# The last matrix product of a three-stage network: half of its K by Strassen's seven products, written transposed

## Chip, cores and metric

The kernel runs on one core of one Trainium2 chip. The metric is the device time of one execution in microseconds (us).

## What is computed

An attention over 2 x 12 heads of 448 tokens, then a two-layer network with a leaky ReLU, then a gated network behind a root-mean-square norm, all in float32:

```python
scores = cap * tanh(q @ k.T / 8 / cap);  attn = softmax(scores);  x = attn @ v    # 2 x 12 x 448 x 64 -> x: 896 x 768
h = x @ w_in;  g = maximum(0.01 * h, h);  x = g @ w_out                            # 768 -> 2048 -> 768
xn = x / sqrt(mean(x * x) + 1e-6) * rms_g
g = xn @ w_gate;  silu = g / (1 + exp(-g));  val = xn @ w_val                      # 768 -> 1536, twice
out = (silu * val) @ w_out2                                                         # 1536 -> 768
```

## The kernel before

Each float32 operand of the large products is split into an upper and a lower part (`hi`, `lo`, of type fp32r), and a product is three matmuls: hi by hi, hi by lo, lo by hi. ScalarE (ACT) copies the upper parts, GpSimd (POOL) or VectorE (DVE) subtracts to make the lower ones. All order is written out by hand, engine by engine, with semaphores; each engine works through its own list and stands still when the head of the list waits.

**Strassen units.** The gate and value products run as 12 units, `s = U1` to `UNITS - 1` (8 to 19), one for each 128 of the 1536 hidden features. A unit computes a 2 x 2 block product (gate and value rows by the two halves of K, times K halves by the two batches) as seven products P1, P5, P7, P6, P3, P2, P4 of 9 matmuls each (`product`, L1345 to L1360: 3 tiles of K by 3 matmuls of 128 x 448), 63 in all. The operands of tokens (`x_hi`, `x_lo`, seven blocks B11, T1, T3, T2, B22, B21, T4 of three tiles) stay for all units. For every weight panel ACT makes `w_hi` (L632), POOL `w_lo` (L518), in a ring of seven slots, so that panel n waits until PE has used panel n - 7. DVE adds weight panels up for P5, P7, P6, P3 (`s_part`, L933 to L942).

**Around PE in a unit.** P3 goes on in the bank of P5, and so waits until DVE has taken P5 out of it (`take_p5`, L955, semaphore `a_done`). `take_p5` adds to P1, which ACT has copied out (`keep_p1`, L638, `p1_kept`). P4 goes on in the bank of P7 and waits for `take_p7` (L961, `a2_done`), P2 waits for `p1_kept`. The rest of the unit on DVE: `take_p6` L965, `value_22` L1162, `gate_sum` L1168, `gate_12` L1172, `gate_11` L1177, `value_21` L1181, and `weighted` (L1188 and L1191), which writes the two tiles of `act_full` (features x tokens, 12 x 2 tiles of 128 x 448). ACT does silu between (L801).

**Last product before.** 504 matmuls at L1516 (`token_tile`): the stationary operand is a 128 x 128 piece of `act_full`, split into `split_hi` and `split_lo` for each of 7 tiles of tokens, the moving one is a row block of `w_out2` (`v2_hi`, `v2_lo`), 384 columns wide (512 and 256 for the last tile). Panels `v2` are split ahead: four during units 13 to 18, the other eight in unit 19 and after. DVE and ACT scale the results (L1262, L854) and SP stores them.

Of the kernel before, what the change touches and what calls it, by code (L numbers as in the profile page):

```python
# [17 lines left out]
def build(nc, qk, v, cap, w_in, w_out, w_gate, w_val, w_out2, rms_g, out, recips):  # L18
    PAIRS, _, QK = qk.shape
    S = out.shape[0] // 2  # L20
# [20 lines left out]
    P1, P5, P7, P6, P3, P2, P4 = range(7)  # L41
# [4 lines left out]
    UNITS = U1 + N2  # L46

# [22 lines left out]
    pe_order += list(range(W_OUT, widx(UNITS, 0)))  # L70
    count = {n: i + 1 for i, n in enumerate(pe_order)}
    assert len(count) == widx(UNITS, 0)

    with ExitStack() as ctx:
# [24 lines left out]
        u2 = [buf(f"u2_{s}", S, F32) for s in range(2)]  # L99
        extra = buf("extra", S, F32)  # L100
        r_bc = buf("r_bc", B * S, F32)
        sq_acc = buf("sq_acc", B * S, F32)
# [28 lines left out]
        EARLY = 4  # L131
        v2_hi, v2_lo, v2_raw = [], [], []
        for where in (RING, SPARE):
            at(where)
            for _ in range(EARLY // 2):
                v2_hi.append(buf(f"v2_hi{len(v2_hi)}", DM, F32R))
                here = place["at"]
                v2_raw.append(buf(f"v2_raw{len(v2_raw)}", DM, F32))
                at(here)
                v2_lo.append(buf(f"v2_lo{len(v2_lo)}", DM, F32R))  # L140
        split_hi, split_lo = [], []
        for where, late, split, part in ((XH, v2_hi, split_hi, "hi"), (XL, v2_lo, split_lo, "lo")):
            at(where)
            split.append(buf(f"split0_{part}", N2 * 128, F32R))
            for k in range(EARLY, N2):
                late.append(buf(f"v2_{part}{k}", DM, F32R))
            split.append(buf(f"split1_{part}", N2 * 128, F32R))
# [19 lines left out]
        v2_in = [sem(f"v2_in{s}") for s in range(EARLY)]  # L167
# [58 lines left out]
        v2_hi_done = sem("v2_hi_done")  # L226
        v2_lo_pool = sem("v2_lo_pool")
        v2_lo_dve = sem("v2_lo_dve")
        v2_lo_half = sem("v2_lo_half")
        split_hi_done = sem("split_hi_done")  # L230
        split_lo_done = sem("split_lo_done")
        rows_done = sem("rows_done")
        evac_act = sem("evac_act")
        evac_dve = sem("evac_dve")
# [112 lines left out]
        def v2_block(k):  # L347

            return (N2 * 128 + (k - EARLY + 1) * DM - 1) // (KH * S)

        def split_block(tt):
            return (N2 * 128 - 1 + tt * (N2 * 128 + (N2 - EARLY) * DM)) // (KH * S)


        v2_pool = list(range(EARLY)) + list(range(EARLY, N2, 2))
        v2_dve = list(range(EARLY + 1, N2, 2))

        def wait_v2_lo(eng, k):
            if k in v2_pool:
                eng.wait_ge(v2_lo_pool, v2_pool.index(k) + 1)  # L360
            else:
                eng.wait_ge(v2_lo_dve, v2_dve.index(k) + 1)

        def pieces_of(tt):
            return [(0, 11), (11, 12)] if tt == 0 else [(0, N2)]

        def pieces_done(tt):
            return sum(len(pieces_of(t)) for t in range(tt))


        def half_cols(tt, half):
            cut = HALF if tt < TT - 1 else 512
            return slice(cut * half, cut if half == 0 else DM)

        def staging(tt, half):
            return (p1 + a_t)[(2 * tt + half) % 4][:, 0:HALF] if tt < TT - 1 else r_bc[:, half_cols(tt, half)]

        def row_bank(tt, half):
            c = half_cols(tt, half)
            return ps[:, (4 + 2 * tt + half) % 8, 0:c.stop - c.start]  # L380

        def unit_of(n):

            if n < W_OUT:
                return n // 7, n % 7
            return U1 + (n - W_GV) // 7, (n - W_GV) % 7

        def w_source(n):

            if W_OUT <= n < W_GV:  # L390
                k = n - W_OUT
                return w_raw[(RAW_OUT + k // 2) % 4][:, cols(k % 2, HALF)]
            s, j = unit_of(n)
            if j in (P1, P2):
# [5 lines left out]
        def v2_source(k):  # L400
            return v2_raw[k][:, :] if k < EARLY else w_raw[(RAW_V2 + k - EARLY) % 4][:, :]
# [5 lines left out]
        def _(sp):  # L407
# [32 lines left out]
            def raw_free(r):  # L440
# [63 lines left out]

        @block.gpsimd
        def _(pool):
# [73 lines left out]
            def value_lo(k):  # L580
                pool.wait_ge(v2_hi_done, k + 1)
                pool.tensor_tensor(v2_lo[k][:, :], v2_source(k), v2_hi[k][:, :].bitcast(F32), ALU.subtract).then_inc(v2_lo_pool, 1)

            def value_lo_half(k, half):
                pool.wait_ge(v2_hi_done, k + 1)
                c = cols(half, HALF)
                lower = pool.tensor_tensor(v2_lo[k][:, c], v2_source(k)[:, c], v2_hi[k][:, c].bitcast(F32), ALU.subtract)
                if half == 1:
                    lower.then_inc(v2_lo_pool, 1)
                else:  # L590
                    lower.then_inc(v2_lo_half, 1)
# [1011 lines left out]
```

## Time and profile before

| | |
|---|---|
| time, median of 3 runs | 575.03 us (574.76 to 576.02) |
| profiled execution: its own time | 574.06 us |
| its span, first to last instruction | 572.3 us |
| PE busy | 567.6 us, 99% |
| weight loads (PEld), DVE, ACT, POOL busy | 493.5, 357.0, 277.6, 271.9 us |
| granted TensorE clock | 1.000 of 2.4 GHz |

1.8 us of the profiled execution's time lie outside its span. PE's busy time counts overlapping matmuls once, so that it says that matmuls follow each other without a gap, not that each is as short as it could be. The rows below are in us from the start of the span.

### The profile page before, as it was taken

To read this page: it belongs to the slowest core of one execution; us is meant where nothing else is said; L and a number is where in the kernel's file an instruction comes from. 1 tells how busy PE (TensorE), PEld (TensorE's weight loads), DVE (VectorE), ACT (ScalarE), POOL (GpSimd) and SP (SyncE) were. 2 spreads that over 40 slices of the span, in tenths; PEclk is the share of its full clock that TensorE was granted. 3 is DMA by queue.
4 is the path that set the end of the run, shared out by engine and by line. 5 is a ranking of instruction groups with operands and counts; after the bars stand their busy time and mean duration, and the time that the engine had idled before them with its cause. 6 is when DMAs were issued, how large, how long until landed. Compare 5 with 4: busy or idle time off the path is not lost.

```text
span 572.3 us, 7765 instructions
## 1 busy us (share of the span) xinstructions
PE 567.6 (99%) x2823; PEld 493.5 (86%) x2823; DVE 357.0 (62%) x484; ACT 277.6 (49%) x453; POOL 271.9 (48%) x236
## 2 busy tenths in 40 slices
PE   8999999999999999999999999999999999999998
PEld 5555655799999999999999999999999999999997
DVE  4479897685555455326974699988788878511120
ACT  6889888236544454437533555333445435311110
POOL 1036373569665633226643487755688855000000
PEclk9999999999999999999999999999999999999999
DMA  6355432213112222120210011611111114000001
GB/s 170 95 173 164 116 102 65 43 49 111 57 55 67 98 85 57 55 56 27 84 55 29 2 55 57 218 58 56 57 56 55 56 60 162 29 27 29 29 27 56
DMA packets 30006, 41.49 MB, mean 73 GB/s; under 512 B 17040, under 2 KB 18832, under 8 KB 29968
## 3 DMA queue, kind: packets, MB, share of 16 engines
q1 hardware_dynamic: 29824, 40.99, 22.9%
q8 instruction: 23, 0.38, 0.3%
q14 instruction: 15, 0.12, 0.1%
q10 hardware_dynamic: 144, 0.00, 0.0%
HBM read 38.15 MB, written 2.80 MB: 72 GB/s over the span
## 4 chain that ended last, share of the span: by engine, by line
PE 98%; DMA 1%; DVE 1%; issue 0%; DVEq 0%
PE ps L1358 45%; PE ps L1425 21%; PE ps L1516 15%; PE ps L1295 10%; PE ps L1283 4%; PE ps L1301 2%; PE ps L1287 2%; DMA qk_raw<-in_qk 1%; PE ps L1477 0%; PE ps L1500 0%; DVE qk_lo L986 0%; DVE qk_lo L991 0%; DVE r_bc L1262 0%; DVE qk_hi L984 0%; DVE capc L999 0%
## 5 line engine op out<-in xcount | busy, mean ns | idle before, releaser
L518 POOL TENSOR_TENSOR w_lo<-w_raw,w_hi 128x384 fp32r<-128x384 f32 x92 | 107.2, 1169 | 133.8 <-ACT w_hi L632 133.5
L1358 PE MATMUL ps<-x_hi,w_hi 128*128 128x448 f32 x420 | 154.2, 367 | 0.0
L1358 PE MATMUL ps<-x_hi,w_lo 128*128 128x448 f32 x420 | 153.4, 365 | 0.0
L1358 PE MATMUL ps<-x_lo,w_hi 128*128 128x448 f32 x420 | 153.4, 365 | 0.0
L518 POOL TENSOR_TENSOR w_lo<-s_sum,w_hi 128x384 fp32r<-128x384 f32 x80 | 89.1, 1121 | 45.1 <-ACT w_hi L632 44.9
L1358 PEld LDWEIGHTS ps<-x_hi,w_hi 128*128 128x128 f32 x420 | 78.9, 188 | 7.6 <-issue 1.1
L1358 PEld LDWEIGHTS ps<-x_hi,w_lo 128*128 128x128 f32 x420 | 78.9, 188 | 6.3
L1358 PEld LDWEIGHTS ps<-x_lo,w_hi 128*128 128x128 f32 x420 | 78.9, 188 | 6.1
L632 ACT ACTIVATE w_hi<-s_sum 128x384 fp32r<-128x384 f32 x80 | 41.6, 523 | 76.9 <-PE ps L1358 67.9
L1295 PE MATMUL ps<-probs,v_ones 128*128 128x448 f32 x144 | 56.8, 542 | 0.0
L632 ACT ACTIVATE w_hi<-w_raw 128x384 fp32r<-128x384 f32 x92 | 47.3, 515 | 7.5 <-PE ps L1358 7.0
L608 ACT ACTIVATE probs<-ps,capc 128x896 f32<-128x896 f32 (+1 forms) x48 | 42.1, 903 | 12.2 <-PE ps L1283 9.7
L1295 PEld LDWEIGHTS ps<-probs,v_ones 128*128 128x128 f32 x144 | 27.0, 189 | 23.1 <-issue 22.6
L1516 PE MATMUL ps<-v_hi,split_lo 128*128 128x384 f32 (+2 forms) x168 | 44.9, 336 | 0.0
L1516 PE MATMUL ps<-v_lo,split_hi 128*128 128x384 f32 (+2 forms) x168 | 44.9, 336 | 0.0
L1516 PE MATMUL ps<-v_hi,split_hi 128*128 128x384 f32 (+2 forms) x168 | 44.9, 336 | 0.0
L615 ACT ACTIVATE probs<-probs,capc 128x1344 f32<-128x1344 f32 (+2 forms) x25 | 41.1, 1643 | 0.8
L1043 DVE TENSOR_TENSOR x_lo<-g,x_hi 128x448 fp32r<-128x448 f32 x32 | 22.1, 737 | 23.7 <-ACT x_hi L664 23.7
L1043 DVE TENSOR_TENSOR ring_lo<-g,ring_hi 128x448 fp32r<-128x448 f32 x32 | 24.6, 813 | 15.2 <-ACT ring_hi L664 15.2
L1516 PEld LDWEIGHTS ps<-v_hi,split_hi 128*128 128x128 f32 x168 | 30.6, 188 | 0.6
L1516 PEld LDWEIGHTS ps<-v_hi,split_lo 128*128 128x128 f32 x168 | 30.6, 188 | 0.5
L1516 PEld LDWEIGHTS ps<-v_lo,split_hi 128*128 128x128 f32 x168 | 30.6, 188 | 0.5
(145 smaller groups left out, 915.8 us busy)
## 6 DMA issues: line engine op xcount, KB each, us to landing
w_raw<-in_w_out SPq DMA_DIRECT2D x24, 384.0 KB, 3.1
w_raw<-in_w_in SPq DMA_DIRECT2D x16, 384.0 KB, 3.6
qk_raw<-in_qk SPq DMA_DIRECT2D x11, 480.0 KB, 4.2
w_raw<-in_w_gate SPq DMA_DIRECT2D x12, 384.0 KB, 3.0
w_raw<-in_w_val SPq DMA_DIRECT2D x12, 384.0 KB, 3.7
v_ones<-in_v SPq DMA_DIRECT2D x12, 224.0 KB, 3.3
recip_row<-recips SPq DMA_DIRECT2D x12, 224.0 KB, 3.4
v_raw<-in_w_out SPq DMA_DIRECT2D x4, 384.0 KB, 6.4
```

The lines of the kernel that those rows point to most:

```text
L518: pool.tensor_tensor(w_lo[:, c], source, w_hi[:, c].bitcast(F32), ALU.subtract).then_inc(w_lo_done, 1)
L608: act.activation(tiles(probs_of(p, i, n), S), ps[:, bank_of(p, i):bank_of(p, i) + n, 0:S], ACT.Tanh, scale=capc[:, 4:5]).then_inc(tanh_don ...
L615: act.activation(c, c, ACT.Exp, scale=capc[:, 2:3], bias=capc[:, 6:7]).then_inc(exp_done, 1)
L632: act.activation(w_hi[:, c], w_source(n), ACT.Copy).then_inc(w_hi_done, 1)
L1043: dve.tensor_tensor(ring(i, b, ring_lo, x_lo), g_tile(2 * f + b), ring(i, b, ring_hi, x_hi).bitcast(F32), ALU.subtract).then_inc(g_lo_done, 1)
L1283: last = pe.matmul(ps[:, bank + h, 0:S], k[HEAD[h], k_c], q[HEAD[h], 0:S], start=(k is hi and q is hi), stop=(k is lo))
L1287: last = pe.matmul(ps[:, bank, 0:S], k[:, k_c], q[:, 0:S], start=(k is hi and q is hi), stop=(k is lo))
L1295: pe.matmul(ps[:, pv_bank(p) + h, 0:S], v_ones[p % 2][:, c:c + 128], probs[p % 2][:, (2 * t + h) * S:(2 * t + h + 1) * S], start=(t == 0), ...
L1301: last = pe.matmul(ps[:, pv_bank(p) + h, 0:S], v_ones[p % 2][HEAD[h], c:c + 128], probs[p % 2][HEAD[h], 2 * MAIN * S:(2 * MAIN + 1) * S], ...
L1358: last = pe.matmul(ps[:, base(s) + BANK_OF[j], 0:S], w[:, w_c], x[:, xs(j, c)], start=(j in (P1, P5, P7, P6) and c == 0 and w is w_hi and ...
L1425: last = pe.matmul(ps[:, ROW_BANK[m] + b, 0:S], w[:, w_c], ring(i, b, beside, in_x), start=(f == 0 and w is w_hi and x == "hi"), stop=(f = ...
L1516: last = pe.matmul(row_bank(tt, half), a[:, c], w[f][:, half_cols(tt, half)], start=(f == 0 and a is hi and w is v2_hi), stop=(f == N2 - 1 ...
```

## The change

1. The last product is computed transposed: the stationary operand is now a panel of `w_out2`, the moving one a tile of `act_full` (448 tokens), the result 768 x 896, and the host turns it. It runs as three units, s = 20, 21, 22, each for two of the six row tiles.
2. In a unit, the first half of K (hidden tiles 0 to 5, `F0 = 6`) is multiplied plainly: 2 rows x 2 batches x 6 tiles x 3 = 72 matmuls (`plain`, four panels PA to PD). The second half (tiles 6 to 11) goes by Strassen's seven products, 63 matmuls. A unit has 135 matmuls and 11 weight panels, three units have 405. Both parts add into the same four banks.
3. Strassen on the token side needs seven blocks of three tiles of activations, made by new code: `z_t1`, `z_t3`, `z_t2`, `z_t4` (sums on DVE), `z_hi` on ACT, `z_lo` on DVE; T1 (for P5) in tiles of its own (`t1_upper`, `t1_lower`), made in units 14 to 19. The splits of the 12 plain tiles are spread over units 11 to 19 (`PLAIN_SPLITS`, `plain_upper` on ACT, `plain_lower_half` on POOL). z tiles and weight panels are begun in unit 19.
4. Results are put together on DVE in two steps each (`result_22`, `_12`, `_11`, `_21`: an addition from the bank, then a multiplication with `r_bc`) and stored as 128 x 448 tiles.
5. In the attention, the product of probabilities and values (`weigh_tile`, `weigh_rest`) loads 65 columns of `v_ones` in place of 128 and writes 65 partitions; DVE reads 65 as before.

```diff
@@ attention
-                    pe.matmul(ps[:, pv_bank(p) + h, 0:S], v_ones[p % 2][:, c:c + 128],
+                    pe.matmul(ps[0:D + 1, pv_bank(p) + h, 0:S], v_ones[p % 2][:, c:c + D + 1],
...
@@ PE: bank_free, the last product
+                if s >= UNITS and j == P1:
+                    pe.wait_ge(u2_done, s - 1)
+                    pe.wait_ge(c22_done, s - 1)
+                elif s >= UNITS and j == P6:
+                    pe.wait_ge(p1_kept, s + 1)
...
+            def plain(s, row, b, half):
...
+                if half == 0:
+                    if (row, b) == (0, 0):
...
+                    elif (row, b) == (0, 1):
+                        pe.wait_ge(a_done, s + 1)
+                    elif (row, b) == (1, 0):
+                        pe.wait_ge(a2_done, s + 1)
+                    else:
+                        pe.wait_ge(u2_done, s + 1)
...
+            for s in range(UNITS, LAST):
+                product(s, P1)
+                product(s, P5)
+                plain(s, 0, 0, 0)
+                plain(s, 0, 0, 1)
+                plain(s, 0, 1, 0)
+                product(s, P7)
+                plain(s, 0, 1, 1)
+                plain(s, 1, 0, 0)
+                product(s, P6)
+                plain(s, 1, 0, 1)
+                plain(s, 1, 1, 0)
+                plain(s, 1, 1, 1)
+                for j in (P3, P2, P4):
+                    product(s, j)
@@ ACT, from unit 19 on
+            s = UNITS
+            keep_p1(s - 1)
+            last_weights(s, P1)
+            t1_upper(2)
+            z_upper(B11)
+            last_weights(s, P5)
+            z_hi(T3, 0)
+            z_hi(T3, 1)
+            last_weights(s, PA, PB)
+            silu(s - 1, 1)
+            last_weights(s, P7)
+            z_hi(T3, 2)
+            silu(s - 1, 0)
+            last_weights(s, PC)
+            z_upper(T2)
+            last_weights(s, P6, PD)
+            keep_p1(s)
...
@@ DVE, end of unit 18, unit 19 and after
+                if s - U1 - F0 in (0, 2, 4):
+                    z_t1((s - U1 - F0) // 2)
+                if s - U1 - F0 in (2, 4):
+                    t1_lower((s - U1 - F0) // 2 - 1)
...
+            def z_t2(c):
+                dve.wait_ge(t3_done, c + 1)
+                dve.wait_ge(z_lo_done, z_count[B11, c])
+                dve.tensor_tensor(z_tile(T2, c), z_tile(T3, c), z_tile(B11, c), ALU.add).then_inc(t2_done, 1)
...
+            def result_21(s):
+                dve.wait_ge(prod_done, count[widx(s, P4)])
+                dve.tensor_tensor(u2[s % 2][:, :], bank(s, BANK_D), u2[s % 2][:, :], ALU.add).then_inc(c21_done, 1)
+                dve.wait_ge(c21_done, s + 1)
+                dve.tensor_tensor(u2[s % 2][:, :], u2[s % 2][:, :], r_bc[:, cols(0)], ALU.mult).then_inc(o_done, 1)
```

What moves is shown by the order of instructions in the built programs. In the rows, `a_t_61` is `a_t[1]`, `u_1_63` is `u2[1]`, `p_0_58` is `p1[0]`, `t_tile` and `t_lo` are T1's tiles, `w_raw_51` a loaded weight panel; line numbers are those of each program.

DVE before, the end of unit 18 (the two `weighted` lines) and the first half of unit 19:

```order
L1188 TENSOR_TENSOR act_full<-a_t_60,sq_68 128x448
L1191 TENSOR_TENSOR act_full<-u_0_62,sq_67 128x448
L955 TENSOR_TENSOR a_t_61<-ps,p_1_59 128x448
L961 TENSOR_TENSOR a_t_61<-ps,a_t_61 128x448
L1201 TENSOR_TENSOR split_lo<-act_full,split_hi 128x1408
L965 TENSOR_TENSOR u_1_63<-ps,p_1_59 128x448
```

DVE in the change, the same place (L1244 is `z_t1`, L1248 `t1_lower`, L1253 `z_t3`, L1267 `z_lo`, L972 and L975 `s_part`, L996 `take_p5`, L1002 `take_p7`):

```order
L1236 TENSOR_TENSOR act_full<-u_0_62,sq_67 128x448
L1244 TENSOR_TENSOR t_tile<-act_full 128x448
L1248 TENSOR_TENSOR t_lo<-t_tile,t_hi_103 128x448
L972 TENSOR_TENSOR s_sum<-w_raw_52 128x384
L975 TENSOR_TENSOR s_sum<-w_raw_51,w_raw_52 128x384
L996 TENSOR_TENSOR a_t_61<-ps,p_1_59 128x448
L1253 TENSOR_TENSOR act_full<-act_full 128x448 x2
L1248 TENSOR_TENSOR t_lo<-t_tile,t_hi_104 128x448
L1267 TENSOR_TENSOR x_lo<-act_full,x_hi 128x448
L1002 TENSOR_TENSOR a_t_61<-ps,a_t_61 128x448
L1267 TENSOR_TENSOR x_lo<-act_full,x_hi 128x448 x2
L1008 TENSOR_TENSOR u_1_63<-ps,p_1_59 128x448
```

Between unit 18's last instruction and `take_p5` of unit 19 there were none and are now four; between `take_p5` and `take_p7` there were none and are four.

DVE in the change, the second half of unit 19 up to `take_p5` of unit 20, the last row (L1211 is `gate_sum`, L1215 `gate_12`, L1230 and L1236 `weighted`, L1258 `z_t2`); before, no instruction of this kind followed, only two pieces of splitting:

```order
L1211 TENSOR_TENSOR sq_68<-ps,u_1_63 128x448
L1215 TENSOR_TENSOR sq_68<-sq_68,r_bc 128x448
L1267 TENSOR_TENSOR x_lo<-act_full,x_hi 128x448
L1230 TENSOR_TENSOR act_full<-a_t_61,sq_68 128x448
L1253 TENSOR_TENSOR act_full<-act_full 128x448
L1220 TENSOR_TENSOR sq_67<-ps,r_bc 128x448
L978 TENSOR_TENSOR s_sum<-s_sum,w_raw_51 128x384
L1267 TENSOR_TENSOR x_lo<-act_full,x_hi 128x448
L1224 TENSOR_TENSOR u_1_63<-ps,u_1_63 128x448
L1236 TENSOR_TENSOR act_full<-u_1_63,sq_67 128x448
L1258 TENSOR_TENSOR act_full<-act_full 128x448 x3
L981 TENSOR_TENSOR s_sum<-w_raw_51,s_sum 128x384
```

From unit 18's last instruction to the third `z_t2` DVE has two instructions of T1's, then 26 of unit 19's list; L996 of unit 20 stands right behind the last row.

ACT in the change, from the second silu of unit 19 to `keep_p1` of unit 20 and beyond (L835 is `z_hi`, L648 `weight_hi`, L656 `keep_p1`):

```order
L819 ACTIVATE sq_67<-sq_67 128x448
L648 ACTIVATE w_hi<-w_raw_54 128x384
L835 ACTIVATE x_hi<-act_full 128x448 x3
L648 ACTIVATE w_hi<-s_sum 128x384
L648 ACTIVATE w_hi<-w_raw_54 128x384
L656 ACTIVATE p_0_58<-ps 128x448
L835 ACTIVATE x_hi<-act_full 128x448 x6
```

The copy of P1 of unit 20 (L656) stands behind the three upper parts of T2, which wait for `z_t2` on DVE. Before, there was no such copy after unit 19's.

## Rows read from the trace of the kernel before

**Rows 1.** The page: busy shares, and slices of the span.

```profile
PE 567.6 (99%) x2823; PEld 493.5 (86%) x2823; DVE 357.0 (62%) x484; ACT 277.6 (49%) x453; POOL 271.9 (48%) x236
...
PE   8999999999999999999999999999999999999998
...
DVE  4479897685555455326974699988788878511120
...
POOL 1036373569665633226643487755688855000000
PEclk9999999999999999999999999999999999999999
```

**Rows 2.** Chain that ended last, 300 to 573: start, length, what.

```profile
348.29 133.16 PE ps L1358 x657
481.45 88.11 PE ps L1516 x504
```

**Rows 3.** DVE's groups, 360 to 470: busy us, mean ns, idle before.

```profile
L1191 DVE TENSOR_TENSOR act_full<-u,sq 128x448 f32<-128x448 f32 x9 | 13.0, 1441 | 0.0
L1172 DVE TENSOR_TENSOR sq<-sq,r_bc 128x448 f32<-128x448 f32 x9 | 11.6, 1292 | 0.3
L936 DVE TENSOR_TENSOR s_sum<-w_raw,w_raw 128x384 f32<-128x384 f32 x8 | 11.1, 1382 | 0.0
L939 DVE TENSOR_TENSOR s_sum<-s_sum,w_raw 128x384 f32<-128x384 f32 x9 | 8.3, 925 | 0.0
L942 DVE TENSOR_TENSOR s_sum<-w_raw,s_sum 128x384 f32<-128x384 f32 x9 | 7.8, 869 | 1.3 <-DVE s_sum L939 0.5
...
L1188 DVE TENSOR_TENSOR act_full<-a_t,sq 128x448 f32<-128x448 f32 x9 | 5.5, 617 | 0.0
...
L933 DVE TENSOR_TENSOR s_sum<-w_raw 128x384 f32<-128x384 f32 x8 | 4.4, 546 | 0.0
```

**Rows 4.** DVE's instructions in order of time: start, length, which.

```profile
450.62 0.61 DVE L965 TENSOR_TENSOR u<-ps,p 128x448 f32<-128x448 f32 x1
451.15 0.61 DVE L1162 TENSOR_TENSOR a_t<-ps,a_t 128x448 f32<-128x448 f32 x1
452.39 0.63 DVE L1168 TENSOR_TENSOR sq<-ps,u 128x448 f32<-128x448 f32 x1 [0.64 <-PE ps L1358]
453.06 1.34 DVE L1172 TENSOR_TENSOR sq<-sq,r_bc 128x448 f32<-128x448 f32 x1
...
458.39 0.55 DVE L933 TENSOR_TENSOR s_sum<-w_raw 128x384 f32<-128x384 f32 x1
458.86 1.38 DVE L936 TENSOR_TENSOR s_sum<-w_raw,w_raw 128x384 f32<-128x384 f32 x1
460.16 0.61 DVE L955 TENSOR_TENSOR a_t<-ps,p 128x448 f32<-128x448 f32 x1
...
469.79 1.44 DVE L1191 TENSOR_TENSOR act_full<-u,sq 128x448 f32<-128x448 f32 x1
```

**Rows 5.** POOL's instructions in order of time.

```profile
458.81 1.01 POOL L518 TENSOR_TENSOR w_lo<-w_raw,w_hi 128x384 fp32r<-128x384 f32 x1 [0.82 <-ACT w_hi L632]
```

**Rows 6.** ACT's instructions in order of time.

```profile
457.77 0.55 ACT L638 ACTIVATE p<-ps 128x448 f32<-128x448 f32 x1 [1.30 <-PE ps L1358]
458.21 0.52 ACT L632 ACTIVATE w_hi<-w_raw 128x384 fp32r<-128x384 f32 x1
```

**Rows 7.** Start of the last product, on PE.

```profile
481.28 0.52 PE L1516 MATMUL ps<-v_hi,split_hi 128*128 128x384 f32 x2
```

**Rows 8.** The end: last matmul, last scaling, last store.

```profile
569.26 0.28 PE L1516 MATMUL ps<-v_hi,split_lo 128*128 128x256 f32 x1
569.58 0.48 DVE L1262 TENSOR_SCALAR r_bc<-ps,rms 128x256 f32<-128x256 f32 x1 [11.97 <-PE ps L1516]
570.09 0.33 SPq L500 DMA_DIRECT2D out<-r_bc  x1
```

**Rows 9.** All stores of the output.

```profile
DMA to landing us min/median/max: 1.7/2.0/3.7
```

**Rows 10.** Chain, 40 to 60: products with the values, one of 12 pairs.

```profile
44.98 4.51 PE ps L1295 x12
49.49 0.95 PE ps L1301 x4
```

**Rows 11.** Weight loads of these products: duration ns min/median/max.

```profile
L1301 PEld LDWEIGHTS ps<-probs,v_ones x48: 182/184/186, 16.6 to 104.3; 64*128 64x128 f32 x48
```

**Rows 12.** The same for L1295.

```profile
L1295 PEld LDWEIGHTS ps<-probs,v_ones x144: 186/190/191, 9.2 to 103.4; 128*128 128x128 f32 x144
```

More of the change, by code:

```diff
@@ L19, in build @@
     PAIRS, _, QK = qk.shape
-    S = out.shape[0] // 2
+    S = out.shape[1] // 2
     B, D, T = 2, 64, 4
@@ L129, in build @@
         SPARE = place["at"]
[L131 to L147, printed above, removed]
+        at(G)
+        act_lo = buf("act_lo", N2 * B * S, F32R)
+        at(RING)
+        plain_ring = buf("plain_ring", 8 * S, F32R)
+        at(SPARE)
+        plain_spare = buf("plain_spare", 4 * S, F32R)
+        T1_AT = place["at"]
+        t1_tile = buf("t1_tile", KH * S, F32)
+        at(T1_AT)
+        t1_lo = buf("t1_lo", KH * S, F32R)
+        at(EXTRA)
+        t1_hi = [buf("t1_hi0", S, F32R)]
+        at(SQ_ACC)
+        t1_hi += [buf(f"t1_hi{k}", S, F32R) for k in (1, 2)]
         ps = ctx.enter_context(nc.psum_tensor("ps", [128, 8, 512], F32))
@@ L364, in pieces_of @@
[L364 to L380, printed above, removed]
+        PLAIN = [(k, b) for k in range(F0) for b in range(B)]
@@ new lines, in z_tile, with t1, z_parts, result @@
+        def z_tile(blk, c):
+            return {B22: act_tile(F0 + KH + c, 1), B21: act_tile(F0 + KH + c, 0), T3: act_tile(F0 + c, 1)}.get(blk, act_tile(F0 + c, 0))
+        def t1(k, c):
+            return k[:, cols(c)]
+        def z_parts(*blks):
+            return [(blk, c) for blk in blks for c in range(KH)]
+        z_all = z_parts(B11, T3, T2, B22, B21, T4)
+        z_count = {part: i + 1 for i, part in enumerate(z_all)}
+        def result(s, kind):
+            return ((1, 1, a_t[s % 2]), (0, 1, sq[1]), (0, 0, sq[0]), (1, 0, u2[s % 2]))[kind]
@@ L578, in _, with plain_lower_half @@
                 weight_lo(widx(U1 + 1, j))
[L580 to L591, printed above, removed]
+            def plain_lower_half(i):
+                k, b = PLAIN[i]
+                pool.wait_ge(plain_hi_done, i + 1)
+                pool.tensor_tensor(plain_lo(k, b), act_tile(k, b), plain_hi(k, b).bitcast(F32), ALU.subtract).then_inc(plain_lo_done, 1)
             for s in range(U1 + 2, UNITS):
@@ new lines, in _ @@
+                if s - U1 - F0 in (2, 4):
+                    t1_lower((s - U1 - F0) // 2 - 1)
+            s = UNITS - 1
+            s_part(s + 1, P5)
+            s_part(s + 1, P7)
+            take_p5(s)
+            z_t3(0)
+            z_t3(1)
+            t1_lower(2)
+            z_lo(B11, 0)
+            take_p7(s)
+            z_lo(B11, 1)
+            z_lo(B11, 2)
+            take_p6(s)
+            value_22(s)
+            z_lo(T3, 0)
+            gate_sum(s)
+            gate_12(s)
@@ new lines, in _ @@
+            z_lo(T3, 1)
+            weighted_1(s)
+            z_t3(2)
+            gate_11(s)
+            s_part(s + 1, P6)
+            z_lo(T3, 2)
+            value_21(s)
+            weighted_0(s)
+            for c in range(KH):
+                z_t2(c)
+            s_part(s + 1, P3)
+            s = UNITS
+            take_p5(s)
+            for c in range(KH):
+                z_lo(T2, c)
+            take_p7(s)
+            for c in range(KH):
+                z_t4(c)
+            for c in range(KH):
+                z_lo(B22, c)
@@ new lines, in _ @@
+            take_p6(s)
+            for blk in (B21, T4):
+                for c in range(KH):
+                    z_lo(blk, c)
+            result_22(s)
+            s_parts(s + 1)
+            result_12(s)
+            result_11(s)
+            result_21(s)
+            for s in range(UNITS + 1, LAST):
+                take_p5(s)
+                take_p7(s)
+                take_p6(s)
+                result_22(s)
+                if s + 1 < LAST:
+                    s_parts(s + 1)
+                result_12(s)
+                result_11(s)
+                result_21(s)
@@ L1589 @@
         "w_val": panels(inputs["moe2_w_val"]),
[L1590 removed]
+        "w_out2": panels(w_out2).reshape(dm // 128, 128, 2, f2 // 2).transpose(0, 2, 1, 3),
         "rms_g": inputs["moe2_rms_g"],
```

367 lines of the change are left out of this document (202 added, 165 removed).

## The prediction

> **What bounds the kernel now.** I began with the page's busy shares and slices [rows 1]. The reader is to see 99% on PE and a 9 in every slice but the first and the last, at a granted clock of 9 (full) throughout: no other engine ends anything for long. The chain that ended last confirms it [rows 2]: units 10 to 19 with the end of unit 9 are one unbroken piece of 657 matmuls in 133.16 us, 0.2027 us each, and the last product one piece of 504 in 88.11 us. So a matmul taken out is worth 0.2027 us, and anything that makes PE stand still is paid in full. DVE has 8s and 9s up to the last product and 0 to 2 in it, POOL 5 to 8 and then nothing [rows 1]: the change puts work on DVE where it was nearly full (units 18 and 19), so I read its list next [rows 3, 4].
>
> Two numbers set DVE's pace. An instruction on 448 columns starts 0.53 us after the one before (450.62, 451.15), one on 384 columns 0.47 (458.39, 458.86) [rows 4]. And an instruction with both inputs in SBUF takes much longer when POOL works: L1191 1.44 us where L1188, of the same form, takes 0.62; L936 1.38 where L933 takes 0.55 [rows 3]. L936 of 458.86 was issued while POOL's L518 ran from 458.81 for 1.01 us [rows 5], and the next instruction started at 460.16 [rows 4], 0.34 after POOL's end: DVE waited for POOL and then did its work. The five such lines of a unit lose 0.82, 0.68, 0.84, 0.38 and 0.32 us against 0.617 and 0.546 [rows 3], 0.61 on average.
> The Trainium skill (SBUF — State Buffer, Who interferes with whom) says that `tensor_tensor` with both inputs in SBUF contends with GpSimd's reads; by that rule the new DVE work, nearly all of this form, is the dearest kind to add beside POOL, and the trace agrees.
>
> **The change, part by part**, against the profiled execution (574.06 us, span 572.3); its time is 0.97 below the median of the runs, 575.03, and I add the difference to the median.
>
> *PE's work.* 504 matmuls become 405 of 448 columns. 405 x 0.2027 = 82.1, against 88.1 [rows 2]: -6.0.
>
> *Where PE waits.* In unit 20 PE does P1, P5 and two plain pieces, 36 matmuls, then needs `a_done`, since the next piece adds to the bank of P5. Unit 20 can start where the last product started, 481.28 [rows 7]; its B11 tiles must be there by then, for which see below. So PE asks for `a_done` at 481.28 + 36 x 0.2027 = 488.6. It is set by `take_p5` of unit 20, which waits for ACT's copy of P1, which stands behind the upper parts of T2, which wait for `z_t2` on DVE. The sum for DVE:
> - unit 18's last instruction ends at 469.79 + 1.44 = 471.2 [rows 4];
> - `z_t1` 0.53, `t1_lower` beside POOL's w_lo about 1.4 (as L1191): 473.1;
> - of unit 19's list 26 instructions to the third `z_t2`: 23 of 448 and 3 of 384 columns, 23 x 0.53 + 3 x 0.47 = 13.6;
> - POOL does six things meanwhile (w_lo of P5, PA, PB, P7, PC and the plain tile 11). Each meets a DVE instruction of the slow form; placing them one by one I get 3.9 in all, 0.65 each, near the average of 0.61. If they cost what these five lines lose spread over all seven panels, 3.04 / 7 = 0.43, it is 2.6; at the dearest line's 0.84, 5.0;
> - instructions that need the result just made start 0.14 later (452.39 to 453.06, where 0.53 would do [rows 4]), four times, with silu about 0.6.
> The third T2 tile is there at 473.1 + 13.6 + 3.9 + 0.6 = 491.2. ACT then copies its last T2 tile (0.44), two weight panels (0.41 each) and P1 (0.55, [rows 6]), `take_p5` takes 0.61 and semaphores about 0.2: 493.9. PE waits 5.3 us (4.0 to 6.4 by the bounds on POOL), and 0.1 to start again.
> Behind `take_p5` DVE has the lower parts of T2; PE wants P6 after 36 more matmuls, 7.3 us on, and they need 3 x 0.53 and one meeting with POOL. Nothing else is late.
>
> *Before unit 20.* `take_p5` of unit 19 ends about 474.6 (473.1 + 0.94 + 0.61); PE, which starts unit 19 at 481.28 - 63 x 0.2027 = 468.5, needs it at 468.5 + 36 x 0.2027 = 475.8. `take_p7` follows two `z_t3`, `t1_lower`, one `z_lo`, two meetings with POOL: about 478.9; P4 needs it at 479.4. The third B11 tile comes after `z_lo` twice more, 1.1 and two meetings: about 481.2; its matmuls come at 481.28 + 6 x 0.2027 = 482.5. So these cost nothing, with 0.5 us to spare at the tightest. If the DVE is later by d, it is d on the whole and not twice, since the 5.3 would shrink by what PE lost before.
>
> *Plain splits and panels.* Twelve ACT copies of 0.44 in nine units where ACT is half idle, and POOL's in place of the `v2` panels it did there: not on the path. The loads are as many bytes as before and a unit ahead. In units 21 and 22 DVE has at most 15 instructions in 135 x 0.2027 = 27.4 us, ACT and POOL 11 panels: PE does not wait. Should a store be late, `take_p5` and `take_p6` of unit 22 wait for one issued a unit before; it lands in 2.0 to 3.7 [rows 9]: covered by 20 us.
>
> *The end.* Before, 2.76 us from the last matmul's end (569.26 + 0.28) to the end of the span. Now: 0.04, addition 0.67 to the next start, multiplication 0.61, issue 0.03, landing 2.0 (the median of 192 KB stores in place of 1.7 for the 128 KB one) [rows 8, 9], and the 0.5 after it: 3.85. +1.1.
>
> *The 65 columns.* L1295 takes 0.376 a record, 12 in 4.51, and L1301's 4 take 0.95 where two such pairs would be 0.75 [rows 10]: up to 0.2 us of weight load is exposed for each of 12 pairs, 2.4 in all. A load of 64 rows takes 184 ns, of 128 rows 190 [rows 11, 12]: rows don't matter, and no row has fewer columns. Bounds: 0 and half of 2.4, -1.2. I take -0.3, nearer to nothing, since the loads' length moved so little with size.
> The Trainium skill (TensorE: Matmul & The Clock Gate, LDWEIGHTS) gives a load as P / 1.2 ns for P columns, rows aside: 107 ns becomes 54, which over 12 to 24 exposed loads is an estimate of 0.6 to 1.3 us, so that the sum would be 0.3 to 1.0 lower than with mine. That rows matter little the trace shows; columns no run here shows.
>
> Sum: -6.0 + 5.3 + 0.1 + 1.1 - 0.3 = +0.2. 574.3 for such an execution, 575.2 as a median.
>
> **Rivals.**
> 1. *POOL costs DVE more* (slower). Place: unit 19's list on DVE. One more meeting is +0.84 at the dearest [rows 3], and at 5.0 in all the wait is 6.4: 575.2 + 1.1 = 576.3; with one more, or with 65 columns worth nothing, 577.2. It decides from +1.0 on DVE's chain. For: every line added to DVE is of the slow form. Against: POOL has long idle times here. 0.28.
> 2. *DVE is quicker than I add up* (faster). With 2.6 for POOL the wait is 4.0, and with -1.2 for the columns 573.0. For: two T1 tiles and the lower parts may fall where POOL stands idle. Against: the five lines of before meet POOL in every unit. 0.15.
> 3. *PE is fed throughout* (faster): the preparation begun a unit sooner does what it says. Then 575.03 - 6.0 + 1.1 - 0.3 = 569.8. It needs the P1 copy 5.3 us sooner, as with eight of DVE's 26 instructions not ahead of it; the order shows all 26. 0.05.
> 4. *The columns are worth it* and the rest is as summed: 574.3, within 0.2% still; in the forecast's case.
>
> **How the numbers follow.** 0.2% is 1.15 us, about what a measurement of this kernel can tell from no change. The forecast's case, 574.0 to 576.2, has 0.52. Rival 1 is slower in nearly all of its 0.28. Rival 2 gives 573.0 to 573.9, rival 3 less: faster 0.20. The range reaches over rivals 1 and 2, 572.9 to 577.4, and leaves out rival 3.
>
> **What would show it.** In the profile of the changed kernel: 405 matmuls in the last product at 0.203 each; one gap on PE of 5 us some 36 matmuls into it, released by `take_p5` (L996), that by ACT's L656, that by DVE's L1258; DVE without a gap from 470 to 491; the slow form at 1.0 to 1.6 us beside POOL; 3.9 us from the last matmul to the end; L1301's four records at 0.85 to 0.95. I am wrong if the gap is under 4 or over 6.5, if PE waits elsewhere in units 19 to 22, or if the products with the values move by over 1.2 us.

## The result, and the profile after

The changed kernel takes 577.89 us (577.45 to 578.95), the kernel before beside it 575.29: 1.0047 times as long, 95% interval 1.0031 to 1.0062. Forecast were 575.2 us and a range up to 577.4. It is slower by 2.6 us, and outside the range.

The profiled execution took 578.34 us, with a span of 576.5. First the page's busy shares and slices, to lay beside [rows 1]:

```profile
PE 565.0 (98%) x2724; PEld 475.6 (82%) x2724; DVE 390.3 (68%) x543; ACT 287.1 (50%) x495; POOL 308.0 (53%) x269
...
PE   8999999999999999999999999999999999699997
...
DVE  4479896595654354336974799988888999681513
...
PEclk9999999999999999999999999999999999899999
```

PE has 99 matmuls fewer, as forecast, and one slice with a 6; in the same slice the granted clock shows an 8, where the kernel before had a 9 throughout. The chain that ended last has the same place in detail (start, length, what):

```profile
349.72 120.40 PE ps L1509 x594
...
491.26 0.62 DVE act_full L1258
...
491.96 0.49 ACT x_hi L835
...
493.94 0.49 ACT w_hi L648
494.44 0.44 ACT p L656
494.87 0.02 issue
494.90 0.64 DVE a_t L996
495.53 0.04 issue
495.58 3.62 PE ps L1686 x9
499.19 1.85 PE ps L1509 x9
501.05 3.69 PE ps L1686 x18
```

Read upward from 495.58, this is the chain that the prediction wrote down: `take_p5` (L996) releases PE, the copy of P1 (L656) releases `take_p5`, and ahead of the copy stand two weight panels and the upper parts of T2, which had waited for `z_t2` (L1258). Read downward, there is something the prediction doesn't have: the nine matmuls behind the stand-still take 3.62 us, while the same form takes 3.69 for eighteen a little later. PE's matmuls in order of time, with the time stood still in brackets:

```profile
489.87 0.37 PE L1686 MATMUL ps<-plain_spare,w_lo 128*128 128x448 f32 x1
495.58 0.74 PE L1686 MATMUL ps<-plain_ring,w_hi 128*128 128x448 f32 x1 [5.34 <-DVE a_t L996]
496.12 0.57 PE L1686 MATMUL ps<-act_lo,w_hi 128*128 128x448 f32 x1
496.49 0.57 PE L1686 MATMUL ps<-plain_ring,w_lo 128*128 128x448 f32 x1
...
498.73 0.46 PE L1686 MATMUL ps<-plain_ring,w_lo 128*128 128x448 f32 x1
499.03 0.36 PE L1509 MATMUL ps<-x_hi,w_hi 128*128 128x448 f32 x1
499.23 0.37 PE L1509 MATMUL ps<-x_lo,w_hi 128*128 128x448 f32 x1
```

From start to start the gap is 5.71 us, of which 0.205 is the matmul's own: PE stands 5.5 us. Behind it the starts lie 0.37 us apart (496.12, 496.49), and 0.20 from 499.03 on. Nine matmuls need 499.03 - 495.58 = 3.45 where they would need 9 x 0.205 = 1.85: 1.6 us more, below called the surcharge. The windows say why (columns: width of the window, busy time of PE with its count, granted clock, share of DMA, GB/s):

```profile
494.00:495.00 1.00, 0.00 (x0) 1.00 0.00 0
495.00:496.00 1.00, 0.42 (x1) 0.76 0.00 0
496.00:497.00 1.00, 1.00 (x4) 0.50 0.00 0
...
498.00:499.00 1.00, 1.00 (x4) 0.53 0.00 0
499.00:500.00 1.00, 1.00 (x6) 1.00 0.00 0
```

The granted clock was 1.00 (2.4 GHz), fell to 0.50 (1.2 GHz) just as PE had stood still for 5.5 us and began again, and was back at 1.00 by 499. The Trainium skill (TensorE: Matmul & The Clock Gate, Why this matters for your kernels) warns that a long enough gap between matmuls in the middle of a kernel puts the clock back to its lower level; by that rule the wait costs more than its own length, and the trace agrees, with 1.6 us on top of 5.5.

The end of the kernel, in order of time:

```profile
572.37 0.36 PE L1509 MATMUL ps<-x_hi,w_lo 128*128 128x448 f32 x1
572.76 0.62 DVE L1296 TENSOR_TENSOR u<-ps,u 128x448 f32<-128x448 f32 x1 [0.46 <-PE ps L1509]
573.42 0.62 DVE L1298 TENSOR_TENSOR u<-u,r_bc 128x448 f32<-128x448 f32 x1
574.07 0.33 SPq L514 DMA_DIRECT2D out<-u  x1
```

From the last matmul's start to the end of the span are 576.5 - 572.37 = 4.15 us, where [rows 8] with the span of 572.3 have 3.0. The weight loads of the products with the values, beside [rows 11, 12]:

```profile
L1432 PEld LDWEIGHTS ps<-probs,v_ones x144: 133/138/138, 9.2 to 103.3; 128*65 128x65 f32 x144
L1438 PEld LDWEIGHTS ps<-probs,v_ones x48: 130/132/134, 16.4 to 104.2; 64*65 64x65 f32 x48
```

**A yardstick for the runs.** Executions of one kernel lie up to 4 us apart (the kernel before: 573.72 to 577.93 in 34). Its three profiles have spans of 572.3, 573.5 and 573.2, and the whole of that difference lies ahead of the last product, whose first matmul starts at 481.28, 482.56 and 482.22. What the last product and the end take is the same in all three. So for each profile I take the span less the start of the last product's first matmul: 572.3 - 481.28 = 91.0 for the kernel before, in all three profiles; 576.5 - 482.71 = 93.8 for the changed one. The difference, 2.8, stands beside that of the medians, 2.6.

### The profile page after: what moved, and what is told of

Read it like the earlier page. It is cut to its first block, busy times and chain, and to the rows that moved or that the text cites. A ratio compares the mean times of both kernels' runs of the same rounds, so it can differ in the third digit from the quotient of the medians.

```text
span 576.5 us, 7775 instructions
## 1 busy us (share of the span) xinstructions
PE 565.0 (98%) x2724; PEld 475.6 (82%) x2724; DVE 390.3 (68%) x543; ACT 287.1 (50%) x495; POOL 308.0 (53%) x269
## 4 chain that ended last, share of the span: by engine, by line
PE 90%; DVE 6%; issue 2%; DMA 1%; ACT 0%; DVEq 0%; ACTq 0%
PE ps L1509 49%; PE ps L1576 20%; PE ps L1432 8%; PE ps L1686 7%; PE ps L1420 3%; PE ps L1438 2%; PE ps L1424 1%; DVE x_raw L911 1%; DMA qk_raw<-in_qk 1%; DVE act_full L1253 0%; DVE x_lo L1267 0%; DMA sums<-x_raw 0%; DVE s_sum L978 0%; DVE sums_eps L917 0%; DVE act_full L1236 0%
## 5 line engine op out<-in xcount | busy, mean ns | idle before, releaser
L538 POOL TENSOR_TENSOR w_lo<-w_raw,w_hi 128x384 fp32r<-128x384 f32 x113 | 131.5, 1169 | 160.9 <-ACT w_hi L648 160.4
L1509 PE MATMUL ps<-x_hi,w_hi 128*128 128x448 f32 x474 | 174.3, 368 | 0.0
L1509 PE MATMUL ps<-x_hi,w_lo 128*128 128x448 f32 x474 | 173.5, 366 | 0.0
L1509 PE MATMUL ps<-x_lo,w_hi 128*128 128x448 f32 x474 | 173.5, 366 | 0.0
L648 ACT ACTIVATE w_hi<-s_sum 128x384 fp32r<-128x384 f32 x92 | 47.8, 523 | 93.9 <-PE ps L1509 68.5
L648 ACT ACTIVATE w_hi<-w_raw 128x384 fp32r<-128x384 f32 x113 | 57.8, 515 | 38.1 <-PE ps L1686 20.7
L1432 PE MATMUL ps<-probs,v_ones 128*65 128x448 f32 x144 | 56.6, 541 | 0.4 <-DVE x_raw L911 0.4
L1432 PEld LDWEIGHTS ps<-probs,v_ones 128*65 128x65 f32 x144 | 19.3, 137 | 30.6 <-issue 29.7
L981 DVE TENSOR_TENSOR s_sum<-w_raw,s_sum 128x384 f32<-128x384 f32 x23 | 25.9, 1124 | 2.5 <-DVE s_sum L978 0.5
L1576 PE MATMUL ps<-ring_hi,w_lo 128*128 128x448 f32 x96 | 27.5, 368 | 0.0
L1576 PE MATMUL ps<-ring_hi,w_hi 128*128 128x448 f32 x96 | 27.5, 367 | 0.0
L1576 PE MATMUL ps<-ring_lo,w_hi 128*128 128x448 f32 x96 | 27.5, 368 | 0.0
```

The lines of the kernel that those rows point to most:

```text
L538: pool.tensor_tensor(w_lo[:, c], source, w_hi[:, c].bitcast(F32), ALU.subtract).then_inc(w_lo_done, 1)
L648: act.activation(w_hi[:, c], w_source(n), ACT.Copy).then_inc(w_hi_done, 1)
L981: dve.tensor_tensor(dst, m1[:, upper], s_sum[:, cols(2, HALF)], ALU.subtract).then_inc(s_done, 1)
L1432: pe.matmul(ps[0:D + 1, pv_bank(p) + h, 0:S], v_ones[p % 2][:, c:c + D + 1], probs[p % 2][:, (2 * t + h) * S:(2 * t + h + 1) * S], start=( ...
L1509: last = pe.matmul(ps[:, base(s) + to, 0:S], w[:, w_c], x, start=(j in (P1, P5, P7, P6) and c == 0 and first), stop=(c == KH - 1 and w is ...
L1576: last = pe.matmul(ps[:, ROW_BANK[m] + b, 0:S], w[:, w_c], ring(i, b, beside, in_x), start=(f == 0 and w is w_hi and x == "hi"), stop=(f = ...
```

## The experiments

Theory: the wait at `a_done` in unit 20, and with it the half clock, turn a gain into a loss. Rivals: the half clock has another origin; the 65 columns or the stages ahead cost something; the end costs more.

**1. Both evacuations early.** ACT copies P1 of unit 20 ahead of unit 19's silu, and VectorE takes the fifth product after the third `z_t3`.

```diff
             last_weights(s, PA, PB)
+            keep_p1(s)
             silu(s - 1, 1)
...
             last_weights(s, P6, PD)
-            keep_p1(s)
...
             weighted_1(s)
             z_t3(2)
+            take_p5(s + 1)
             gate_11(s)
...
             s = UNITS
-            take_p5(s)
```

> The changed kernel with ACT's copy of P1 of unit 20 moved ahead of silu, and DVE's take_p5 of unit 20 moved behind the third z_t3 of unit 19. Theory A (PE's 5.5 us gap is the queue ahead of copy and take_p5, and the half clock of 3.4 us after it, worth 1.7, is a consequence of the gap): both go, 577.9 - 5.5 - 1.7 = 570.7 us, between 570 and 572, and no matmul at the lower clock. Theory B (DVE's whole list is the bound, whichever instruction PE waits for): the wait turns up one step later, at P6, for the lower parts of T2, and 575 us or more is left.

573.26 us, 0.9971 (0.9957 to 0.9986): faster than both kernels. The wait at `a_done` is gone, but two others are in its place:

```profile
496.45 0.44 PE L1686 MATMUL ps<-plain_ring,w_hi 128*128 128x448 f32 x1 [1.28 <-issue]
502.89 0.47 PE L1686 MATMUL ps<-plain_ring,w_hi 128*128 128x448 f32 x1 [0.66 <-DVE u L1008]
```

The matmuls ahead of them started at 494.80 and 501.86, so PE stands 1.45 and 0.83 us, for `take_p7` and `take_p6` of unit 20, which stand on VectorE behind the lower parts of T2 and B22. Their order is the same in the changed kernel, where the long wait and the slow matmuls behind it gave VectorE time for them. The granted clock of this stretch is 1.00, so these two stand-stills left it alone, and all ten executions have a mean of 0.998 to 1.0. The two waits, 2.3 us together, are nearly all of what the time lies above theory A's 570.7. Theory B put what is left at 575 or more, and at the lower parts themselves.

**2. The copy alone early**: of experiment 1 only the first part.

> Only ACT's copy of P1 moved, take_p5 stays behind the three z_t2 and one s_part on DVE. Theory A: a_done comes some 2 us sooner (take_p5 at about 492.7 instead of 494.9 in the profile), the gap is 3.5 us; 577.9 - 2.0 = 575.9 if the clock falls all the same, 574.2 if a gap of 3.5 us does not bring it down. Theory B: the same as theory A here.

576.36 us, 1.0024 (1.0007 to 1.0041), near the 575.9 that go with a fall of the clock. PE stands 3.9 us instead of 5.5 (491.53 to 495.65, start to start), but the clock falls sooner with respect to PE's restart:

```profile
493.00:494.00 1.00, 0.00 (x0) 1.00 0.00 0
494.00:495.00 1.00, 0.00 (x0) 0.68 0.00 0
495.00:496.00 1.00, 0.35 (x1) 0.50 0.00 0
...
501.00:502.00 1.00, 1.00 (x6) 0.91 0.00 0
```

Half clock lasts to 501, so more matmuls pay for it: in this execution the shorter wait has the larger surcharge, 2.6 us. It is the slowest of the ten, though (579.37 us). By the medians, 576.36 and 577.89, the copy alone is worth 1.5 us, about the 1.6 by which the wait got shorter, so on the whole the surcharge stayed.

**3. The wait filled.** In the changed kernel, 24 matmuls whose result is overwritten stand ahead of the waiting piece.

```diff
+                if s == UNITS:
+                    pe.wait_ge(c21_done, s - 1)
+                    for _ in range(24):
+                        pe.matmul(ps[:, base(s) + BANK_D, 0:S], w_hi[:, 0:128], t1_hi[0][:, :], start=True, stop=True)
                 plain(s, 0, 1, 0)
```

> The changed kernel with 24 matmuls of no use (448 columns, 24 x 0.203 = 4.9 us) on PE in the gap, into the bank that P7 starts anew afterwards; nothing else moved. Theory A (the clock falls because PE stands still): PE's real gap is under 1 us, the clock stays at its upper level, and the time is 577.9 - 1.7 = 576.2 us. Rival C (the plain matmuls after the gap are slow in themselves, by their operands or bank): 9 of them still take 0.37 us each, and 577.9 stays.

576.93 us, 1.0026 (1.0009 to 1.0043). The stretch on PE:

```profile
488.01 5.03 PE L1700 MATMUL ps<-t_hi,w_hi 128*128 128x448 f32 x24
493.57 0.47 PE L1686 MATMUL ps<-plain_ring,w_hi 128*128 128x448 f32 x1 [0.52 <-DVE a_t L996]
493.88 0.36 PE L1686 MATMUL ps<-act_lo,w_hi 128*128 128x448 f32 x1
494.08 0.37 PE L1686 MATMUL ps<-plain_ring,w_lo 128*128 128x448 f32 x1
```

Nothing useful is done sooner, the piece that waits for `a_done` starts 12.9 us after the last product began, as in the changed kernel, and yet the matmuls behind it start 0.20 apart, at a granted clock of 1.00. PE itself stands only 0.7 us. The yardstick gives 92.35 against 93.8. The medians, 576.93 and 577.89, are only 1.0 us apart and their intervals overlap. For the clock the run speaks by its profile and by the mean granted clock of all nine executions, 0.998 to 1.0; the changed kernel has 0.993 to 0.997 in each of its six.

**4. The 65 columns alone** in the kernel before.

```diff
-pe.matmul(ps[:, pv_bank(p) + h, 0:S], v_ones[p % 2][:, c:c + 128],
+pe.matmul(ps[0:D + 1, pv_bank(p) + h, 0:S], v_ones[p % 2][:, c:c + D + 1],
```

> The kernel before with the 65 columns alone. From the profile of the changed kernel, in which PE was 0.57 us ahead by 60 us and only 0.03 by 101: 575.0 to 575.3 us, nothing that can be measured. Rival: the saving stays and the time is 574.6 or less. It also shows whether the 1.6 us that units 2 to 7 took longer in the changed kernel's profile (0.2067 us a matmul in place of 0.2027) belong to this edit: then 576.5 or more.

575.35 us, 0.9996 (0.9982 to 1.0011): between -1.0 and +0.6 us, no effect that can be told from none, and the last product stays at 91.0.

**5. All three evacuations early.** From experiment 1, `take_p7` and `take_p6` of unit 20 come after the first lower part of T2 and of B22 instead of after the third.

```diff
-            for c in range(KH):
-                z_lo(T2, c)
+            z_lo(T2, 0)
             take_p7(s)
+            for c in range(1, KH):
+                z_lo(T2, c)
...
-            for c in range(KH):
-                z_lo(B22, c)
+            z_lo(B22, 0)
             take_p6(s)
+            for c in range(1, KH):
+                z_lo(B22, c)
```

> On top of both evacuations made early: in unit 20 VectorE takes the seventh product after the first T2 lower part instead of after the third, and the sixth after the first B22 lower part instead of after the third. The version before it still had TensorE standing 1.45 us at 494.8 (for the seventh product's evacuation, which ended at 496.35) and 0.83 us at 501.9 (for the sixth's, which ended at 502.84). Theory 1 (only these two waits are left): both go, 2.3 us less than 573.26, so 571.0 us (570.4 to 571.8), span 569.0, granted clock 1.0 before the tail. Rival (the split parts that are now 0.6 and 1.2 us later are waited for in their turn, by the products P6, P3, P2 or P4): one of the waits comes back further on, 572.3 to 573.3 us.

571.69 us, 0.9940 (0.9924 to 0.9956). One of the two waits is gone; of the other is left

```profile
502.55 0.48 PE L1688 MATMUL ps<-plain_ring,w_hi 128*128 128x448 f32 x1 [0.64 <-DVE u L1008]
```

with 0.8 us of stand-still (the matmul ahead started at 501.54). `take_p6` started at 501.88, although P6 had ended at about 500.3: it stood behind the B22 part, which ran from 500.53 for 1.43 us beside POOL.

**6. The kernel before, held up once.** GpSimd does five dependent operations on an idle buffer when token tile 2 is done, and PE waits for them before tile 3. Nothing else in the kernel waits.

```diff
+            pool.wait_ge(rows_done, 6)
+            for k in range(5):
+                at_least(pool, pause, k)
+                pool.tensor_tensor(extra[:, 0:HALF], extra[:, 0:HALF], extra[:, 0:HALF], ALU.mult).then_inc(pause, 1)
...
                 elif tt in (2, 3):
                     pe.wait_ge(act_done, 2 * N2)
+                    if tt == 3:
+                        pe.wait_ge(pause, 5)
```

> The kernel before, with TensorE held up once in its last product, between the third and the fourth token tile, by five dependent GpSimd operations on an idle buffer (1.06 us each plus about 0.2, so about 5.4 us); nothing else waits. Nothing is left out. Theory 1 (a stand-still of this length costs the stand-still and then a stretch at half the granted clock, 3.4 or 6.8 us of it, at 0.373 instead of 0.2027 us a matmul): 575.2 + 5.4 + 1.5 to 3.1 = 582.1 to 583.7 us, mean granted clock 0.993 to 0.997, and matmuls of twice the usual pitch right behind the gap. Rival (the half clock in the changed kernel came from something else in its place, not from the stand-still): 580.6 us, clock 1.0.

582.89 us, 1.0134 (1.0117 to 1.0151), a mean granted clock of 0.994 in all four executions, against 0.999 to 1.0 in the twelve of the kernel before. PE's matmuls (two to a row) around the stand-still:

```profile
519.58 0.51 PE L1521 MATMUL ps<-v_hi,split_lo 128*128 128x384 f32 x2
...
526.28 0.98 PE L1521 MATMUL ps<-v_hi,split_hi 128*128 128x384 f32 x2 [6.19 <-issue]
527.06 0.84 PE L1521 MATMUL ps<-v_lo,split_hi 128*128 128x384 f32 x2
527.70 0.84 PE L1521 MATMUL ps<-v_hi,split_lo 128*128 128x384 f32 x2
...
531.17 0.51 PE L1521 MATMUL ps<-v_hi,split_lo 128*128 128x384 f32 x2
```

The gap came out longer than planned, 6.53 us from start to start (the last matmul ahead of it started at 519.75). Behind it a matmul has 0.32 us (527.06, 527.70 for two) and from 531 on again 0.175. From the first to the last matmul of the product are 96.40 us against 87.98: 8.4, of which 6.35 stand-still and 2.05 surcharge. So the half clock comes from the stand-still and not from the changed kernel's work.

**7. The same with two operations.**

> The same with two GpSimd operations, a stand-still of about 2.3 us; nothing is left out. Stand-stills of 1.45 and 0.83 us left the clock alone in the version with both evacuations early, those of 3.9 and 5.5 us did not. Theory 1a (2.3 us is still free of a fall): 577.5 us, clock 1.0. Theory 1b (it falls here as well, in all or some executions): 578.5 to 580.6 us, clock 0.993 to 0.998.

577.70 us, 1.0051 (1.0033 to 1.0069). PE stands 2.1 us, the product is 2.13 longer, the granted clock 1.00 from before the pause to the last matmul; six of seven executions have a mean of 1.0, the seventh 0.997 and the longest time, 580.38. That one looks like a fall, though no profile shows it; at this length it is at most the exception.

**8. The changed kernel again.**

> The changed kernel itself once more, beside the others on the same chip. Theory 1: 577.9 us (577.3 to 578.5), every execution at a mean granted clock of 0.993 to 0.997, where the kernel before has 0.999 to 1.0. On the pitch of 0.2067 instead of 0.2027 us in units 2 to 7 (127 to 207 us: 388 matmuls where most profiles have 396): if it varies from execution to execution, this profile shows either; if it belongs to the changed kernel's program, it shows 388 again, and the kernel carries 1.6 us more that no step of the prediction has.

578.10 us, 1.0056 (1.0035 to 1.0077). All twelve timed executions of the changed kernel, these and the first six, have a mean clock of 0.993 to 0.997. The stand-still is 5.5 us again, but the clock fell earlier in it:

```profile
493.00:494.00 1.00, 0.00 (x0) 0.70 0.00 0
...
499.00:500.00 1.00, 1.00 (x4) 0.50 0.00 0
500.00:501.00 1.00, 1.00 (x6) 0.88 0.00 0
```

Here the surcharge is 90.25 - 89.65 = 0.6 us larger than in the first profile, 2.2 in all.

**9. P6 first.** From experiment 5, `take_p6` one operation sooner, ahead of the first B22 part.

```diff
-            z_lo(B22, 0)
             take_p6(s)
+            z_lo(B22, 0)
```

> As the version with all three evacuations early, with the sixth product of unit 20 taken one VectorE operation sooner, ahead of the first B22 lower part (1.43 us) instead of behind it. That version had one stand-still left, 0.81 us at 501.5, for the sixth product's evacuation, which began at 501.88 although the product had ended at about 500.3. Theory 1: the stand-still goes, 571.7 - 0.8 = 570.9 us (570.2 to 571.6). Rival (the B22 lower part that is now 0.6 us later is asked for at once by the product that follows): 571.7 us, with a gap at another line.

570.80 us, 0.9922 (0.9894 to 0.9951): 4.45 us faster than the kernel before. The chain has no wait from 400 to the end of the matmuls; its beginning:

```profile
399.99 85.95 PE ps L1511 x424
485.94 5.54 PE ps L1688 x27
491.48 1.82 PE ps L1511 x9
493.30 3.69 PE ps L1688 x18
496.99 1.82 PE ps L1511 x9
```

Its product, 82.51 us from first to last matmul, is what 405 matmuls take when nothing waits.

**10 to 12. Both kernels once more, two profiles of the one before and one of the changed.** Units 2 to 7, in the first layer of the network, differ between the two profiles, in a part that the change doesn't touch. The window 127 to 207 of the changed kernel (PE, PEld, DVE, ACT, POOL):

```profile
127.00:207.00 80.00, 80.00 (x388) 72.48 (x387) 42.45 (x62) 39.81 (x83) 51.90 (x48) 1.00 0.23 76
```

and of the kernel before:

```profile
127.00:207.00 80.00, 80.00 (x396) 73.93 (x395) 41.94 (x61) 41.33 (x87) 52.23 (x48) 1.00 0.24 80
```

Eight matmuls fewer, at a granted clock of 1.00 in both, are 1.6 us.

> The kernel before itself, one profile. In units 2 to 7 (127 to 207 us) two patterns of pitch have shown: 396 matmuls (mean 0.2027 us; the kernel before, and four others) or 388 (0.2067; the changed kernel twice, and three others). If it is a matter of the execution, either may show here; if of the program, 396 again. The last product lasts 87.98 us from its first to its last matmul in either case.

> The same once more: execution or program, as in the look ahead of it.

> The changed kernel, one more profile: 388 matmuls in 127 to 207 us for the third time if the slower pitch belongs to its program, 388 or 396 if it is a matter of the execution. Last product 89.5 to 90.5 us from its first to its last matmul, with a stand-still of 5.5 us at unit 20 and half the granted clock behind it.

575.34, 575.00 and 579.53 us. The changed kernel's third last product takes 89.95 us from first to last matmul, with a stand-still of 5.52 us and half the granted clock behind it, as expected. The kernel before has 395 or 396 in its three profiles, the changed one 388, 388 and 389. Of the others, experiments 1, 3, 4, 6 and 9 have 395 or 396, experiments 2, 5 and 7 have 388 or 389. Three and three look like a matter of the program. Against that stands that the timed executions don't show it: experiments 5 (388) and 9 (396) lie 0.9 us apart by their medians, and their last products alone differ by 83.41 - 82.51 = 0.9; experiment 7 (389) is 2.5 above the kernel before, its pause 2.1, where a slower pitch would add 1.6. And the profiled executions with 388 or 389 lie 0.45 to 3.0 us above the median of their kernel, all of them, those with 395 or 396 between 2.1 below and 0.5 above, as they would if it were a matter of the execution. What sets the pattern stays open. The result doesn't need it: see the sum below.

All of them by the yardstick (span less the start of the last product's first matmul, less the 91.0 of the kernel before), beside the difference of the medians:

| kernel | yardstick | difference | medians |
|---|---|---|---|
| changed | 576.5 - 482.71 = 93.8 | +2.8 | +2.6 |
| changed, again | 577.1 - 482.67 = 94.4 | +3.4 | +2.9 |
| 1, both early | 571.3 - 482.13 = 89.2 | -1.8 | -1.9 |
| 2, copy early | 577.6 - 484.37 = 93.2 | +2.2 | +1.2 |
| 3, filled | 573.0 - 480.65 = 92.35 | +1.35 | +1.7 |
| 4, 65 columns | 573.6 - 482.57 = 91.0 | 0.0 | +0.15 |
| 5, all early | 570.9 - 483.36 = 87.5 | -3.5 | -3.5 |
| 6, long pause | 581.6 - 482.18 = 99.4 | +8.4 | +7.7 |
| 7, short pause | 576.8 - 483.65 = 93.15 | +2.15 | +2.5 |
| 9, P6 first | 568.8 - 482.11 = 86.7 | -4.3 | -4.45 |

The third profile of the changed kernel gives 577.7 - 483.60 = 94.1, +3.1. Differences of the medians are uncertain by 0.8 to 1.7 us; each follows the last product and the end alone about within that. So what the change does ahead of the last product, the columns and the splits spread over units 11 to 19, costs or gains nothing that these runs can tell.

## Why the prediction was wrong

Its sum was +0.2, and measured were +2.6.

**"PE waits 5.3 us (4.0 to 6.4 by the bounds on POOL)"** was right: 5.5. Shifted by the 1.43 us by which the product began later in this profile, the forecast has PE ask at 490.0 (the piece ahead ended at 490.07), the third T2 tile ready at 492.6 (492.9), `a_done` at 495.3 (495.5). The count of VectorE's instructions and the price of meeting POOL bore it out (3.9 us forecast, about 4.1 in the trace), and VectorE had no gap of over 0.2 us between 471 and 491.

**"and 0.1 to start again" is the step that failed.** It prices the restart and no more, as if PE went on at its old speed. Behind the 5.5 us the granted clock was at 0.50 and the surcharge was 1.6 us, 2.2 in the next profile, 1.9 in the third (89.95 - 82.51 - 5.52). Experiment 6 makes it out of nothing but a stand-still, experiment 3 takes it away with the wait for `a_done` left in place. The kernel before has no stand-still near that long (no two of its matmuls start more than 0.9 us apart), so its trace had no row for it; that was a cost to bound, and I left it at nothing. The upper bound of the range, 577.4, has no share for it either: it is 576.3 with one more meeting at 0.84 and the columns at nothing, 0.3. Rival 1 has "or" between these two, which is a slip: without the meeting, columns worth nothing give 576.6 and not 577.2.

**"405 x 0.2027 = 82.1, against 88.1: -6.0"** was 0.5 too good. The 0.2027 is that of the gate and value units (120.40 / 594). In the last product the Strassen pieces take 9.15 for 45, 0.203 each, and the plain ones 5.54 for 27, 0.205 each; together it is 82.51 against 87.98 in experiment 9: -5.5.

**The end** was forecast at +1.1 and came to 4.15 - 3.0 = +1.15. Its store landed after 1.9 us.

**The 65 columns**, -0.3 with bounds 0 and -1.2: a load got shorter by a quarter, 138 ns instead of 190, and L1438's four take 0.90 us as forecast, yet alone they give -1.0 to +0.6. By the Trainium skill (TensorE: Matmul & The Clock Gate, LDWEIGHTS) a load of 65 columns is 53 ns shorter than one of 128, and the trace agrees with that difference, at 52, but not with the lengths themselves, 190 and 138 ns where the page gives 107 and 54; the estimate made from it, 0.6 to 1.3 us, isn't excluded below 1.0 and isn't shown either.

The sum with what was measured: -5.5 + 5.5 + 1.6 to 2.2 + 1.15 + 0 to -0.3 = +2.5 to +3.3; measured +2.6 and +2.9.

Of the rivals, the first (POOL costs more) had the sign and not the cause: VectorE lost to POOL about what was forecast. The third, PE fed throughout at 569.8, was right as a price: with the evacuations in another order it is 570.8, of the missing 1.0 the pitch is 0.5 and the columns, which gave nothing measurable, 0.3. It said that the copy would have to come 5.3 us sooner, and experiments 1, 5 and 9 show that this takes moves of four single operations, two of which only matter once the long wait is gone.

## What to carry to other kernels

If a forecast has TensorE stand still for several microseconds where it was never idle, add a term for matmuls at half the granted clock behind the gap (here 1.6 to 2.6 us on waits of 3.9 to 6.35). Where one engine both takes products out and prepares operands, put each evacuation at the place in its list where the product ends, not behind a group of preparations: moving four single operations turned +2.6 us into -4.45. Under a long wait lie shorter ones, so after taking one away look for the next.

## What was not expected of the hardware

- How far into a stand-still the clock falls varies with the same program: the half level was first seen 0.1 us before PE's restart in one profile of the changed kernel, 2.2 us before it in the next and 2.9 in the third, with equal stand-stills of 5.5 us. The surcharge was 1.6, 2.2 and 1.9 us. The shorter stand-still of 3.9 us in experiment 2 paid more, 89.05 - 82.51 - 3.9 = 2.6 us.
- What the surcharge goes by, in these profiles, is how long the half level lasts past PE's restart, and not the length of the stand-still: 3.4, 4.7 and 4.0 us in the three profiles of the changed kernel, 5.5 in experiment 2 and 4.4 in experiment 6, with surcharges of 1.6, 2.2, 1.9, 2.6 and 2.05, each 0.46 to 0.48 of that time.
- Stand-stills of 0.8, 1.45 and 2.1 us left the clock at 1.00 in the profiles; 3.9, 5.5 and 6.35 us did not.
- At half the granted clock a 448-column matmul took 0.37 us instead of 0.205, and one of 384 columns 0.32 instead of 0.175, so 1.8 times and not twice.
- Five dependent GpSimd operations held PE for 6.35 us where 1.06 us each was expected, and two for 2.1. Four of the five took 0.83 us, 0.9 from one start to the next; the third took 2.4, in a stretch in which VectorE's 1.76 us `split_lo` ran. GpSimd too pays for a meeting, not only VectorE.
- The two patterns of pitch in units 2 to 7 (388 or 396 matmuls in 80 us, at full granted clock), whose cause is open.
